# The last chunk's hidden product ahead of the output products, and the moving operands of the f32r products 64 bytes off a multiple of 256

## The reference

```python
# attention with a window of n_local = 96 keys, n_global = 8 global keys and a linear distance bias
a = exp(scores - max); a = a / (sum(a) + 1e-09); attn = a @ v
# first gated product, causal convolution of 5 taps
gate_pre = sum(conv_w[k] * xp[:, k:k+S, :] for k in range(5))
x = (sigmoid(gate_pre) * (x @ w_val)) @ w_out
# second gated product, 1024 hidden features, centred convolution of 3 taps
h = maximum(x @ w_in, 0.0)
conv_out = sum(conv_w[k] * hp[:, k:k+S, :] for k in range(3))
out = (h * sigmoid(conv_out)) @ w_out
```

## Time and profile before

| | |
|---|---|
| time of the kernel before | 276.95 us, median of 3 runs (276.44 to 277.86) |
| the profiled execution's own time | 277.47 us |
| its span in the trace | 275.7 us |
| granted PE clock | 1.00 of full speed over the span |
| PE busy | 268.2 us (97%), 1574 records |
| PE's weight loads | 211.3 us (77%) |
| DVE busy | 185.7 us (67%) |
| ACT busy | 158.7 us (58%) |
| HBM read, written | 18.37 MB, 3.15 MB |

### The profile page before, as it was taken

One profiled execution on the slowest core, in us unless ns is written; L12 is line 12 of the kernel. 1 busy time (PEld: TensorE's weight loads), 2 busy tenths in 40 slices (PEclk: granted clock), 3 DMA queues, 4 the chain that ended last, 5 costly groups with the idle time before them and its releaser, 6 DMA issues.

```text
span 275.7 us, 4496 instructions
## 1 busy us (share of the span) xinstructions
PE 268.2 (97%) x1574; PEld 211.3 (77%) x1574; DVE 185.7 (67%) x457; ACT 158.7 (58%) x362; POOL 36.3 (13%) x63
## 2 busy tenths in 40 slices
PE   8999999999999999999999999999999999997995
PEld 7544478888788888888888888888888888776884
DVE  0487388878898992798950897688503579999200
ACT  1141588889999982753553407675234577873410
POOL 1011017777133230000000000000000000000000
PEclk9999999999999999999999999999999999999999
DMA  6999625545652000000000000000030000000421
GB/s 200 367 376 330 258 56 183 180 122 163 218 157 76 4 2 0 5 2 0 0 0 0 2 0 0 1 2 0 0 140 14 0 0 1 2 0 0 152 86 66
DMA packets 12152, 21.83 MB, mean 79 GB/s; under 512 B 1760, under 2 KB 2272, under 8 KB 12000
## 3 DMA queue, kind: packets, MB, share of 16 engines
q1 hardware_dynamic: 10976, 20.52, 22.5%
q10 hardware_dynamic: 1152, 1.01, 1.1%
HBM read 18.37 MB, written 3.15 MB: 78 GB/s over the span
## 4 chain that ended last, share of the span: by engine, by line
PE 81%; DVE 12%; ACT 5%; issue 1%
PE ps L530 16%; PE ps L532 16%; PE ps L531 16%; PE ps L414 9%; PE ps L501 7%; PE ps L461 6%; PE ps L479 6%; DVE hgB L1109 4%; ACT prob L671 3%; DVE hgA L1109 2%; PE ps L487 2%; PE ps L429 2%; DVE hglA L1122 2%; DVE hgA L1116 1%; DVE hgB L1116 1%; PE ps L425 1%
## 5 line engine op out<-in xcount | busy, mean ns | idle before, releaser
L671 ACT ACTIVATE prob<-prob,low 128x256 f32<-128x256 f32 (+1 forms) x96 | 46.0, 484 | 4.3 <-DVE low L927 4.3
L530 PE MATMUL ps<-gh,Wh 128*128 128x512 f32 x96 | 37.3, 389 | 0.0
L531 PE MATMUL ps<-gl,Wh 128*128 128x512 f32 x96 | 37.3, 389 | 0.0
L532 PE MATMUL ps<-gh,Wl 128*128 128x512 f32 x96 | 37.3, 389 | 0.0
L785 ACT ACTIVATE h<-ps 128x512 f32<-128x512 f32 x24 | 14.4, 598 | 37.9 <-PE ps L532 37.9
L1109 DVE SCALAR_TENSOR_TENSOR hgA<-h,cw,hgA 128x512 f32<-128x512 f32 x32 | 21.9, 747 | 19.2 <-ACT hgA L797 19.2
L952 DVE SCALAR_TENSOR_TENSOR g<-xT,cw,g 128x512 f32<-128x512 f32 x48 | 32.8, 744 | 2.2 <-ACT g L710 2.2
L927 DVE CUSTOM_DVE_ANT_0 prob<-ps,bias 128x256 f32<-128x256 f32 x80 | 30.0, 413 | 2.6 <-PE ps L461 2.6
L530 PE MATMUL ps<-hghA,w2h 128*128 128x512 f32 x64 | 25.2, 393 | 0.9 <-DVE hglA L1122 0.9
L531 PE MATMUL ps<-hglA,w2h 128*128 128x512 f32 x64 | 24.9, 390 | 0.0
L532 PE MATMUL ps<-hghA,w2l 128*128 128x512 f32 x64 | 24.9, 389 | 0.0
(11 more groups left out here) (92 smaller groups left out, 511.0 us busy)
## 6 DMA issues: line engine op xcount, KB each, us to landing
q_rows<-in_q SPq DMA_DIRECT2D x12, 256.0 KB, 4.3
kW<-in_k SPq DMA_DIRECT2D x12, 256.0 KB, 4.3
v_own<-in_v SPq DMA_DIRECT2D x12, 256.0 KB, 3.0
out<-xT SPq DMA_DIRECT2D x5, 512.0 KB, 2.9
w<-in_w SPq DMA_DIRECT2D x8, 256.0 KB, 10.1
v_win<-in_v SPq DMA_DIRECT2D x10, 192.0 KB, 3.0
prob<-in_wval SPq DMA_DIRECT2D x1, 1024.0 KB, 9.5
win<-in_win SPq DMA_DIRECT2D x1, 1024.0 KB, 11.8
```

The costliest lines, as they stand in the source:

```text
L530: pe.matmul(out, w_hi, x_hi, start=first, stop=False)
L531: pe.matmul(out, w_hi, x_lo, start=False, stop=False)
L532: return pe.matmul(out, w_lo, x_hi, start=False, stop=final)
L671: act.activation(part, part, ACT.Exp, scale=-1.0, bias=low[:, t % 2, i:i + 1], accum_out=total[:, t % 2, i:i + 1]).then_inc(exp_done, 1)
```

## The change

Two things change, and no instruction is added or taken away.

**The order around hid(2).** PE runs hid(2) directly behind hid(1), and out(0), out(1), out(2) come last. Since hid(2) may now have its operands written while hid(1) still reads `gh` and `gl`, chunk 2 gets a pair of its own, `gh_last` and `gl_last`, laid over the start of `xT`. The waits follow: `split_g(2, ...)` no longer waits for hid(1), chunk 1 uses the `hgB` set and chunk 2 the `hgA` set instead of the other way round, out(1) writes the PSUM banks 0 to 3 and out(2) the banks 4 to 7. ACT's and DVE's orders are rewritten to fit.

**The addresses.** Pads are added and resized. The weights `Wh`, `Wl`, `wvh`, `wvl`, `w2h`, `w2l` stay on a multiple of 256 bytes; the first elements of `xh`, `xl`, `gh`, `gl`, `gh_last`, `gl_last`, `hghA`, `hglA`, `hghB`, `hglB` lie 64 bytes behind one. The steps inside them are the same, so all 720 f32r matmuls read weights from a multiple of 256 and moving elements from 64 behind one. The operands of the float32 products stay on multiples of 256.

```diff
+        sb("x_to_256_bytes", [P, 32])
+        over_x = ExitStack()
+        sb("beside_gh_last", [P, 16], where=over_x)
+        gh_last, gl_last = sb("gh_last", [P, CT, N], f32r, over_x), sb("gl_last", [P, CT, N], f32r, over_x)
+        over_x.close()
         xT = sb("xT", [P, CT, B, XROW])
...
-        sb("to_256_bytes", [P, 48])
+        sb("to_256_bytes", [P, 16])
         over_W = ExitStack()
+        sb("beside_hghB", [P, 16], where=over_W)
...
+        sb("W_to_256_bytes", [P, 64])
...
+        sb("beside_hghA", [P, 16], where=over_val)
...
+        sb("beside_xh", [P, 16])
...
-        sb("h_to_256_bytes", [P, 40])
+        sb("beside_gh", [P, 40 + 16])
         gh, gl = sb("gh", [P, CT, N], f32r), sb("gl", [P, CT, N], f32r)

-        hgh, hgl, hg = (hghA, hghA, hghB), (hglA, hglA, hglB), (hgA, hgA, hgB)
+        hgh, hgl, hg = (hghA, hghB, hghA), (hglA, hglB, hglA), (hgA, hgB, hgA)
+        ghs, gls = (gh, gh, gh_last), (gl, gl, gl_last)
...
-        OB = lambda c, m: ps[:, (0 if c == CHUNKS - 1 else 4) + m, :]
+        OB = lambda c, m: ps[:, (0 if c == 1 else 4) + m, :]
...
             hid(1)
+            hid(2)
             pe.wait_ge(w2l_done, FT)
             out(0, range(CT))
-            hid(2)
             out(1, range(CT))
...
             def split_g(c, j):
-                if j == 0 and c > 0:
-                    act.wait_ge(h_mm, FT * c)
+                if j == 0 and c == 1:
+                    act.wait_ge(h_mm, FT)
...
                 if gg == 0 and c == 0:
                     act.wait_ge(v_mm, CT * CHUNKS)
                 elif gg == 0 and c == 1:
+                    act.wait_ge(h_mm, FT * CHUNKS)
+                elif gg == 0:
                     act.wait_ge(o_mm, CT)
-                elif gg == 0:
-                    act.wait_ge(h_mm, FT * CHUNKS)
```

More of the change, by code:

```diff
@@ L68, in program @@
         raw_over_W = ExitStack()
-        sb("below_hgB", [P, FT, N], where=raw_over_W)
+        sb("below_hgB", [P, FT * N + 16], where=raw_over_W)
         hgB = sb("hgB", [P, FT, N], where=raw_over_W)
@@ L78, in program @@
         raw_over_val = ExitStack()
-        sb("below_hgA", [P, FT, N], where=raw_over_val)
+        sb("below_hgA", [P, FT * N + 16], where=raw_over_val)
         hgA = sb("hgA", [P, FT, N], where=raw_over_val)
@@ L86, in program @@
         xh, xl = sb("xh", [P, CT, N], f32r), sb("xl", [P, CT, N], f32r)
+        sb("xl_to_256_bytes", [P, 48])
         over_g = ExitStack()
@@ L598, in part @@
                         cols = slice(m * P, (m + 1) * P)
-                        last = product(HB(m), Wh[:, k, cols], Wl[:, k, cols], gh[:, k, :], gl[:, k, :], k == 0, k == CT - 1)
+                        last = product(HB(m), Wh[:, k, cols], Wl[:, k, cols], ghs[c][:, k, :], gls[c][:, k, :], k == 0, k == CT - 1)
                     if ks[-1] == CT - 1:
@@ L622, in out @@
                         elif k == 0 and c == 1:
+                            pe.wait_ge(relu_done, FT * CHUNKS - 3 + m)
+                        elif k == 0:
                             pe.wait_ge(o_free, m + 1)
-                        elif k == 0:
-                            pe.wait_ge(relu_done, FT * CHUNKS - 3 + m)
                         cols = slice(m * P, (m + 1) * P)
@@ L725, in split_g @@
             def split_g(c, j):
-                if j == 0 and c > 0:
-                    act.wait_ge(h_mm, FT * c)
+                if j == 0 and c == 1:
+                    act.wait_ge(h_mm, FT)
                 act.wait_ge(g_mul, CT * c + 2 * j + 2)
-                act.activation(gh[:, 2 * j:2 * j + 2, :], g[:, 2 * j:2 * j + 2, :], ACT.Copy).then_inc(gh_done, 1)
+                act.activation(ghs[c][:, 2 * j:2 * j + 2, :], g[:, 2 * j:2 * j + 2, :], ACT.Copy).then_inc(gh_done, 1)
             with act.If(banded(act)):
@@ L837, in _ @@
             gates2(0, 0)
+            split_g(2, 0)
+            split_g(2, 1)
             relu(1, 2)
@@ L846, in _ @@
             high2(0, 2)
+            relu(2, 0)
             gates2(0, 3)
-            split_g(2, 0)
-            split_g(2, 1)
             high2(0, 3)
[L852 to L855, removed]
+            for gg in range(1, 4):
+                relu(2, gg)
             first_tap2(1, 0)
-            relu(2, 1)
             first_tap2(1, 1)
             gates2(1, 0)
-            relu(2, 2)
-            high2(1, 0)
             first_tap2(1, 2)
             gates2(1, 1)
-            relu(2, 3)
-            high2(1, 1)
+            high2(1, 0)
             first_tap2(1, 3)
             gates2(1, 2)
+            high2(1, 1)
+            gates2(1, 3)
+            high2(1, 2)
+            high2(1, 3)
+            act.wait_ge(xl_later, CT * 2)
             first_tap2(2, 0)
-            high2(1, 2)
-            gates2(1, 3)
+            copy_out(0, 0)
+            copy_out(0, 1)
             first_tap2(2, 1)
+            copy_out(0, 2)
+            copy_out(0, 3)
             gates2(2, 0)
-            high2(1, 3)
             first_tap2(2, 2)
@@ L1025, in gated1_low @@
                 two = slice(2 * j, 2 * j + 2)
-                dve.tensor_tensor(gl[:, two, :], g[:, two, :], gh[:, two, :].bitcast(f32), ALU.subtract).then_inc(gl_done, 1)
+                dve.tensor_tensor(gls[c][:, two, :], g[:, two, :], ghs[c][:, two, :].bitcast(f32), ALU.subtract).then_inc(gl_done, 1)
             with dve.If(banded(dve)):
@@ L1151, in _ @@
             gated2(0, 0)
[L1152 to L1159, removed]
             gated1_low(2, 0)
             gated1_low(2, 1)
-            low2(0, 3)
[L1163 to L1186, removed]
+            low2(0, 0)
+            for gg in (2, 3):
+                taps2(0, gg)
+                gated2(0, gg - 1)
+                low2(0, gg - 1)
+            gated2(0, 3)
+            low2(0, 3)
+            for c in (1, 2):
+                taps2(c, 0)
+                taps2(c, 1)
+                gated2(c, 0)
+                taps2(c, 2)
+                low2(c, 0)
+                gated2(c, 1)
+                taps2(c, 3)
+                low2(c, 1)
+                gated2(c, 2)
+                gated2(c, 3)
+                low2(c, 2)
+                low2(c, 3)
 def kernel(**inputs):
```

## The result

The changed kernel takes 276.03 us (median of 15 runs, 275.58 to 277.1), the kernel before in the same comparison 277.57 (276.44 to 278.55). The ratio is **0.9949, 95% interval 0.9935 to 0.9963**: 1.4 us or half a per cent faster. The forecast was 266.0 us, with a range from 265.2 to 274.6, so the time lies outside. The profiled execution's span went from 275.7 to 273.9 us.

The account below looks back on a forecast made before the run. PE's own matmuls were taken to bound the kernel: 277.47 us of the profiled execution less 3.3 (order) and 7.8 (addresses) gave 266.4, as a median 265.9, stated as 266.0. Range 265.2 to 274.6 us.

Parts of the forecast that it names:

- PE's matmuls bound the kernel, 226.7 ns each, with 3.3 us of stalls: PE's 720 f32r matmuls set the time; waits for `low2` in out(1) and out(2) lose 3.3 us, which the order recovers.
- The order's slacks: Around hid(2) and the out products: operands and banks ready before PE wants them; smallest slack 1.1 us, at tile 4 of hid(2).
- The addresses, -7.8 us: On all 720 f32r matmuls: 64 bytes' distance between weights and moving operand removes the 10.8 ns excess, at best -7.8 us.
- the three bounds: For the address change: -7.8 us if the excess goes whole, 0 if it belongs to f32r, +7.8 if collisions double.
- Rival 2: f32r matmuls: the new distance collides more; with another 10.8 ns each the kernel takes 281.4 us; chance 0.12.
- threshold, 4.6 ns: Added cost per f32r matmul, a spacing above 231.3 ns, from which the kernel ends slower than before.
- Rival 1: Whole kernel: the order alone counts and addresses change nothing; 273.7 us; chance 0.31.
- Rival 3: At tile 4 of hid(2): a new PE wait for relu(2, 0) replaces the old ones; 277 us; chance 0.07 in full.
- mild form: The third of Rival 2 counted as still faster by over 0.5% despite longer f32r steps.
- 32 clocks: The excess per f32r matmul as the last line states it; if inherent to f32r, the address term is nothing.

Follow-up runs that it names:

- order_only: The changed kernel with the pads taken back, all f32r operands on multiples of 256 bytes: 274.56 us, ratio 0.9897 to the kernel before.
- spacing: Small kernel without the computation: PE alone runs groups of 24 matmuls with shifted operand starts; 227 ns at equal starts, 229 with the moving operand 64 bytes off.
- addresses_only: The kernel before with only the pads added, moving f32r operands 64 bytes behind a multiple of 256: 278.97 us, ratio 1.0051.
- spacing2: Small kernel like `spacing` with more distances, columns and weights; no distance other than zero under 229 ns at 512 columns and 128 columns of weights.
- spacing3: Small kernel of f32r groups at equal starts, operands read in other ways: 216 ns with one moving element repeated, 451 with every second element.
- relu_late: `order_only` with the pair relu(2, 0) moved on ACT behind chunk 0's last high2: 277.15 us, ratio 0.9966 to the kernel before.
- all_64: `order_only` with every tensor moved by 64 bytes, so both f32r operands start 64 behind a multiple of 256: 274.09 us, ratio 0.9882.

## Why the prediction was wrong

- **PE's matmuls bound the kernel, 226.7 ns each, with 3.3 us of stalls:** right. The order alone took 3.4 us off the span, at steps of 226.7 ns.
- **The order's slacks:** right. `gl_last` was predicted done at 178.9 and PE wanted it at 182.05; in `order_only` the `low2` behind it starts at 178.66. Bank 0 was to be free at 191.8 and wanted at 192.9; there the first ReLU starts at 190.94, ends at about 191.5, and PE starts tile 4 at 192.85. Moving the ReLU pair behind two more steps of ACT cost 2.1 us, which shows the slack by experiment.
- **The addresses, -7.8 us:** this is the step that failed, where the prediction says "I take the excess for a collision of these two streams [...] 64 bytes' distance moves them apart" and its sum has the best of the three bounds. No run shows the term, 10.8 ns less on each matmul: the steps went from 226.7 to 228.9 ns with the pads. The 10.8 ns were the author's estimate; what the rows show is an f32r step of 512 columns 10.7 ns longer than a float32 record of 256 (226.7 against 216), and `spacing` shows the same against bfloat16. The measured term is +1.6 us by the steps (+1.4 by the ratio of `addresses_only`). That the excess comes with 512 fresh f32r elements in the time of 256 was right, shown by the matmul that reads each of 256 elements twice at 216 ns. That equal starts cause it was not: for matmuls of this size they are the cheapest of all distances tried (227 ns against 229 and more), and 11 ns over 216 are the least that any distance leaves. Whether a collision of two streams is behind it at all stays open. The trace had one distance only, and the argument went from "the excess has to do with fetching" to "another address removes it" without a row.
- **Rival 2** named the sign, and that a distance of 64 bytes makes the step longer, at a price five times too high (that the streams collide more is not shown): 2.2 ns a matmul at 64 bytes instead of 10.8. Its threshold, 4.6 ns, holds: 2.2 ends faster than before, 6.7 (128 bytes) ends slower.
- **Rival 1**, that addresses change nothing, is not what happened, though its 273.7 us are nearer to 276.0 than the forecast: the distance between weights and moving operand changes f32r's steps from 227 to as much as 237 ns. bfloat16 and float32 took 216 and 429 ns in `spacing` with and without the one offset tried, 64 bytes.
- **Rival 3**'s 277 us is the nearest number of all, by luck: no new wait came.
- **The range**: the chances gave 0.12 to rival 2, and a third of that to its mild form, a loss smaller than the order's gain, which is the case that came; the range left it out. 274.6 to 277 was the gap between rivals that were each priced at one value only.
- **Slips that change nothing above:** PE's last slice in the earlier trace rows is a 5, not 7 to 9; the range's upper end adds 0.9 us to rival 1, where the text allows 0.7; a third of 0.12 is 0.04, which makes 0.85 and not 0.84; and the last line gives the excess as 32 clocks, a count that no run shows, where the sum has 10.8 ns.

## What to carry to other kernels

An unexplained excess in one form of an instruction is not yet a gain: before it is booked, ask for a row in which the edit's own variable has another value, and if there is none, a kernel of 24 matmuls a group gives it in one run. For f32r matmuls of 512 columns by 128 columns of weights keep weights and moving operand at the same place within 256 bytes (0, 32, 64 and 128 were good, 227 to 229 ns, 16 was not, 233); with fewer columns or fewer weights the small kernels show no gain from it (120 ns at equal starts against 118 at 64 bytes with 256 columns, 230 against 228 with 64 columns of weights). The version with the order alone, 0.9897, beats both kernels. A product pulled ahead of others, to let slow engines work under it, was worth the stalls behind it (3.3 us, of which the trace shows all), as long as the bank reuse ahead of it keeps its slack.

## What the runs showed of the hardware

- An f32r matmul of 512 columns by 128 columns of weights costs 227 ns at equal starts (233 with both operands 16 bytes off a multiple of 256), 229 at 64 bytes' distance, 231 to 234 at most others and 237 with the moving operand 4 bytes off (`spacing`, `spacing2`); every second element costs 451, one element over and over or each element twice 216 (`spacing3`). At 448 columns and fewer, 64 bytes cost nothing: 201 ns against 202 at equal starts with 448 columns, 118 against 120 with 256.
- In `relu_late` PE stood still for 2.12 us and had been busy for all of the 80 us from 110 to 190; 1.5 us after it went on, its steps went from 234 ns (227 before the wait) to 427 for about 3.4 us; the granted clock was 0.57 from 196 to 200 us. That cost 8 x 0.2 = 1.6 us besides the wait. Of its 12 executions eight had a mean clock of 1.000 and spans from 273.9 to 275.8 us, four a mean of 0.992 to 0.994 and spans from 275.8 to 277.1, against none of the 4 of `order_only`. So a wait of this length seems to take the clock with it at times, but that is not shown alone to be the cause: one of the 6 executions of `all_64`, which has no such wait in its trace, and two of the 23 of the kernel before in that comparison had means of 0.992 to 0.994 too, with spans over 3 us above the others' median. The longest stall of the kernel before (1.64 us more than a step) did not lower the clock in the trace.
